# Loading w1 by SBUF rows (80 and 48 of 128) instead of by thirds of every row

## What is computed

```
# 1. linear attention with decay; B=4, H=8, S=768, D=48
cur = einsum('bhd,bhe->bhde', u * k_t, v_t)
y_t = einsum('bhd,bhde->bhe', r_t, state + cur)
state = w * state + einsum('bhd,bhe->bhde', k_t, v_t)
# 2. soft mixture of experts; x is 3072 x 384, phi 384 x 32, E=8 experts of 4 slots
logits = x @ phi
d = softmax over tokens;  c = softmax over slots
slot_input = (d.T @ x)                       # 8 x 4 x 384
slot_out[e] = relu(slot_input[e] @ w1[e]) @ w2[e]   # w1[e] 384 x 1024, w2[e] 1024 x 384
x = c @ slot_out
# 3. feed-forward; w_in 384 x 2048, w_out 2048 x 384
out = elu(x @ w_in) @ w_out
```

## Time and profile before

| what | value |
|---|---|
| median of 3 runs | 394.32 us (394.05 to 395.26) |
| profiled execution | 392.18 us |
| its span | 390.4 us |
| PE busy | 374.2 us, 96% |
| PEclk | 9 in all 40 slices |
| DMA queue of SP | 82368 packets, 50.21 MB, 43.1% of 16 engines |

### The profile page before, as it was taken

One profiled execution on the slowest core, in us unless ns is written; L12 is line 12 of the kernel. 1 busy time (PEld: TensorE's weight loads), 2 busy tenths in 40 slices (PEclk: granted clock), 3 DMA queues, 4 the chain that ended last, 5 costly groups with the idle time before them and its releaser, 6 DMA issues.

```text
span 390.4 us, 11439 instructions
## 1 busy us (share of the span) xinstructions
PE 374.2 (96%) x4373; PEld 333.0 (85%) x4373; DVE 267.6 (69%) x512; ACT 219.6 (56%) x498; POOL 103.3 (26%) x136
## 2 busy tenths in 40 slices
PE   6898999999889999999999999999999999999996
PEld 3787898989775454589999999999999999999996
DVE  4787788778767620699867767667777667776671
ACT  2896778777772131588564446444644464455441
POOL 7797777777640000355200000000000000000000
PEclk9999999999999999999999999999999999999999
DMA  7989899999999999920020002000200020002002
GB/s 152 254 151 186 199 234 233 227 255 254 235 303 426 430 432 403 373 64 2 0 83 1 2 0 81 0 0 0 81 0 0 0 81 0 0 0 82 2 2 81
DMA packets 87280, 51.80 MB, mean 133 GB/s; under 512 B 77776, under 2 KB 83024, under 8 KB 85200
## 3 DMA queue, kind: packets, MB, share of 16 engines
q1 hardware_dynamic: 82368, 50.21, 43.1%
q10 hardware_dynamic: 4880, 1.16, 1.4%
HBM read 45.86 MB, written 4.72 MB: 130 GB/s over the span
## 4 chain that ended last, share of the span: by engine, by line
PE 79%; DMA 10%; SPq 3%; issue 3%; ACT 3%; DVE 1%; POOL 1%; DVEq 0%; POOLq 0%; ACTq 0%
PE psum L976 17%; PE psum L978 17%; PE psum L977 17%; PE psum L911 6%; DMA w_out_raw<-in_moe_w_out_dram 4%; PE psum L603 4%; DMA r_raw<-in_r_dram 3%; PE psum L643 3%; PE psum L826 3%; PE psum L686 3%; PE psum L667 2%; PE psum L656 2%; PE psum L696 2%; DMA v_sb<-in_v_dram 1%; PE psum L703 1%
## 5 line engine op out<-in xcount | busy, mean ns | idle before, releaser
L978 PE MATMUL psum<-w_out_hi,elu_lo 128*128 128x384 f32 x372 | 125.8, 338 | 0.0
L976 PE MATMUL psum<-w_out_hi,elu_hi 128*128 128x384 f32 x372 | 125.7, 338 | 0.0
L977 PE MATMUL psum<-w_out_lo,elu_hi 128*128 128x384 f32 x372 | 125.3, 337 | 0.0
L1405 ACT ACTIVATE exp_h<-psum 128x512 f32<-128x512 f32 x96 | 57.6, 600 | 97.3 <-PE psum L911 97.0
L1246 DVE SCALAR_TENSOR_TENSOR elu<-psum,neg_part 128x512 f32<-128x512 f32 x96 | 66.3, 690 | 57.1 <-ACT neg_part L1392 57.1
L977 PEld LDWEIGHTS psum<-w_out_lo,elu_hi 128*128 128x128 f32 x372 | 69.8, 188 | 3.9
L976 PEld LDWEIGHTS psum<-w_out_hi,elu_hi 128*128 128x128 f32 x372 | 70.4, 189 | 0.0
L978 PEld LDWEIGHTS psum<-w_out_hi,elu_lo 128*128 128x128 f32 x372 | 69.9, 188 | 0.0
L1238 DVE TENSOR_TENSOR elu_lo<-elu,elu_hi 128x512 fp32r<-128x512 f32 x96 | 66.3, 691 | 0.6
L1280 ACT ACTIVATE scores<-ident_wide,bonus 128x128 f32<-128x128 f32 x192 | 58.8, 390 | 5.0 <-DVE bonus L1028 4.9
L1392 ACT ACTIVATE neg_part<-exp_h 128x512 f32<-128x512 f32 x96 | 60.0, 626 | 1.7 <-DVE elu L1246 1.3
(11 more groups left out here) (155 smaller groups left out, 403.6 us busy)
## 6 DMA issues: line engine op xcount, KB each, us to landing
w<-in_moe_w_dram SPq DMA_DIRECT2D x8, 1536.0 KB, 13.6
w_sb<-in_moe_w_dram SPq DMA_DIRECT2D x8, 1024.0 KB, 6.3
out_dram<-out_sb SPq DMA_DIRECT2D x24, 192.0 KB, 1.9
w_sb<-in_moe_w_dram SPq DMA_DIRECT2D x8, 512.0 KB, 6.2
w_out_raw<-in_moe_w_out_dram SPq DMA_DIRECT2D x4, 768.0 KB, 15.7
r_raw<-in_r_dram SPq DMA_DIRECT2D x12, 192.0 KB, 3.2
r_raw<-in_r_dram SPq DMA_DIRECT2D x24, 96.0 KB, 3.4
w_in_sb<-in_moe_w_in_dram SPq DMA_DIRECT2D x1, 2304.0 KB, 19.4
```

Source lines behind the costliest of these rows:

```text
L976: pe.matmul(acc, hi, w_out_hi[:, f, :], start=(f == 0), stop=False)
L977: pe.matmul(acc, hi, w_out_lo[:, f, :], start=False, stop=False)
L978: m = pe.matmul(acc, lo, w_out_hi[:, f, :], start=False, stop=(f == KF2 - 1))
L1405: act.activation(exp_h[:, f % 2, :], banks[4 + f % RING][:, :], ACT.Exp).then_inc(exp_done, 1)
```

## The change

The pieces of w1 are cut across the other dimension. In the chunks a piece is now SBUF rows 0 to 79, whole (80 x 12 KB, 960 KB); at the head and in the last chunk it is rows 80 to 127, whole (48 x 12 KB, 576 KB). Number and order of the DMAs and every wait stay as they are; `w1_sb` and its readers are unchanged.

```diff
-            def load_w1(experts, thirds):
+            def load_w1(experts, rows):
 
                 for e in experts:
-                    sp.dma_start(w1_sb[:, e * KD + thirds.start:e * KD + thirds.stop, :], w1_dram[e][:, thirds, :]
-                                 ).then_inc(w1_loaded, 16)
+                    sp.dma_start(w1_sb[rows, e * KD:(e + 1) * KD, :], w1_dram[e][rows, :, :]).then_inc(w1_loaded, 16)
...
                     if not first and not last:
-                        load_w1([2 * (c - 1) + g], slice(0, 2))
+                        load_w1([2 * (c - 1) + g], slice(0, 5 * P // 8))
                     if last and g == 0:
-                        load_w1(range(2, E), slice(2, KD))
+                        load_w1(range(2, E), slice(5 * P // 8, P))
...
-            load_w1(range(2), slice(2, KD))
+            load_w1(range(2), slice(5 * P // 8, P))
```

## The result

The changed kernel takes 424.76 us (median of 6 runs, 421.82 to 425.31), the kernel before 394.19 us in the same comparison: the ratio is 1.080, 95% interval 1.074 to 1.085. The prediction said 413 us, within 393 to 424. The direction was right, and so was the reason given for it, that rows matter; the loss is 30.6 us, not 18.7, and just outside the range.

What follows compares the result with a forecast made beforehand. The prediction took the DMA queue, from the chunks' first load to w_out, to bound the feed-forward's start. Last chunk +11.2, chunks +6.0 and +0.5, head +1.0 gave +18.7 us on 394.3: 413 us, range 393 to 424.

Steps and rivals of the forecast that it cites:

- What bounds the kernel: From the chunks' first load to w_out: the feed-forward starts when the DMA queue has been worked off.
- Rows matter: Loads of w1 covering fewer SBUF rows run slower than their bytes, +18.7 us in sum; chance 0.62.
- The G_T moves: Sign from the kernel before: SBUF-to-SBUF moves on 32 rows, whose packets took 1.7 times as long as their bytes.
- Theory 1: Rows share fixed paths into SBUF; a load is as slow as the path with the most rows.
- Last chunk, +11.2: Six 48-row pieces of w1 in the last chunk take 19.9 us against 8.7, delaying w_out's landing by +11.2 us.
- the factor for 48 rows: In the last chunk and at the head, 48-row loads take 2.4 times their time by bytes, at most 2.67.
- Chunks, +6.5: 80-row pieces in the chunks: six from 48 us on cost +6.0 us, the two before 48 us +0.5 us.
- Head, +1.0: Two 48-row pieces delay chunk 1's k and r loads by 3.7 us, mostly covered by free DMA time: +1.0 us.
- What is late next: In the last chunk w1 lands late and PE stands about 5 us at line 826, not adding to the sum.
- Rows don't matter: Rival for all w1 pieces: only bytes and packet length count, 392.9 to 394.3 us; chance 0.20.
- The engines even it out: Rival: free engines go on to other loads; chunks lose nothing, last chunk only part, +2 to +7 us; chance 0.12.
- Worse than the bound: Rival: head pieces make PE stand in chunk 1, or more than two engines meet on rows: over 424 us; chance 0.06.

Runs made afterwards that it cites:

- e2_alternate: Changed kernel, but w1 cut into every second row (even rows in the chunks, odd rows at the head and in the last chunk): 395.05 us, ratio to before 1.0055.
- e1_halves: Changed kernel, but w1 cut into rows 0-63 in the chunks and rows 64-127 at the head and in the last chunk: 420.84 us, ratio to before 1.070.
- e6_mirror: Changed kernel, but odd experts mirrored: rows 48-127 in the chunks, 0-47 at the head and in the last chunk: 421.26 us, ratio to before 1.071.
- e4_first_two: Kernel before, with whole rows for w1's experts 0 and 1 alone (80 in chunk 1, 48 at the head): 401.23 us, ratio 1.0225.
- e5_last_six: Kernel before, with whole rows for w1's experts 2 to 7 alone (80 in chunks 2 to 4, 48 in the last chunk): 417.55 us, ratio 1.064.
- e3_quarter: Changed kernel, but w1 cut into rows 0-95 in the chunks and rows 96-127 at the head and in the last chunk: 414.12 us, ratio to before 1.053.

## Why the prediction was right in kind and wrong in size

**What bounds the kernel.** Right. The loss appears in full at w_out's landing (29.7 us), and nothing behind it moved.

**Rows matter (0.62).** Right, and shown: e2_alternate and e1_halves differ only in which rows, and by 25.8 us. The G_T moves had been a true sign, although they don't read HBM. That the rows act where they are written, and not where they are read, rests on those moves and on w_out's 396 GB/s, not on an experiment of its own. Theory 1 is the rule that the prediction weighed, "SBUF — State Buffer", section "Door 1: The DMA port swizzle", of the Trainium skill. The runs agree with it where it says that rows 0-63 reach no more ports than rows 0-31 do: 768 KB on 64 rows against 384 KB on 32 took 7.7 against 4.7 us as a pair. They agree, too, with the section "Can I just issue two DMAs to hit both halves?" of the same page of the Trainium skill, by which two loads on different halves don't run beside each other: e6_mirror saved a tenth. They don't test the page's map row by row.

**Last chunk, +11.2, measured +17.5.** The step that failed most is the factor for 48 rows. It was set at 2.4, with 2.67 as its upper bound; measured were 1.37 us a packet, 2.95 times w2's. The bound was the ratio of the rows, 128 to 48; counting 8 rows on the fullest path for either load gives the same number. It supposes that a full path is never idle. The beat of three in the DMA row looks like engines released in groups, which would leave gaps; why the bound was passed was not tested. The factor makes 24.2 us instead of 19.9, +4.3 us. The other 2.0 us are not resolved; the chunk piece ahead of the six was issued only 2.9 us before them (117.10 and 119.95 us) instead of 4.2 and was itself slower, so more of it stood in line ahead of them. The Trainium skill's figures, too, had given 21.7 us for the six by the estimate in the prediction; measured were 24.2, and the measurement decides.

**Chunks, +6.5, measured +7.9.** An interval between pieces grew from 9.66 to 10.98 us on average, +1.3 instead of +1.0, but the last one, to the six pieces, shrank from 4.2 to 2.9 us: from the third piece's issue to the six it is +5.1 us, where the prediction had +6.0. v's landing behind the piece, 6.8 us, was forecast as 6.5 or more. What was wrong is that the two pieces before 48 us would find cover: they cost 2.8 us together, not 0.5 (first to third issue 23.55 us instead of 20.73). e4_first_two shows the same with the other six as before, 23.5 us.

**Head, +1.0, measured +4.3.** The same error in a larger form. I took some 4 us of idle DMA time as cover, but that time did not lie where the delayed loads were: POOL stood 4.4 us for k in the changed kernel, and PE stood 3.66 us in the middle of one group of matmuls at line 642, at 23.4 us. e5_last_six, with the head as before, has its first chunk piece back at 35.67 us. The other traces follow the rows of the two pieces at the head: 36.95 us with 96-127 (e3_quarter), 37.16 with every second row (e2_alternate), 41.51 with 64-127 (e1_halves), 42.44 with 80-127 and 0-47 (e6_mirror). PE's stop comes with the late ones: 3.1 us in e4_first_two, 5.0 in e1_halves and 4.5 in e6_mirror, always after 22 of 32 matmuls; e2_alternate, e3_quarter and e5_last_six have none there. Beside it the granted clock fell: 0.83 in the window from 13.5 to 34 us, where it had been 1.00; one group of eight matmuls at line 602, 1.02 us long at the full clock, took 1.90 us after PE's stop. No experiment here separates the stop's share from the late k's.

**What is late next.** Right in kind: line 825 started at w1's landing (151.77 us instead of 128.0), and that did not add to w_out's delay. But PE stood only 0.85 us there, not about 5, since it had already stood 7.48 us in line 702, which the prediction did not have.

**Rivals.** "Rows don't matter" is out by e1_halves against e2_alternate, and what e2_alternate measured, 395.05 us, is the case in which only bytes and packets count: there the longer packets brought nothing that can be seen. "The engines even it out" is out by e6_mirror. "Worse than the bound", given 0.06, is what the time says, by the head, which is one of the ways it named, and by a price above the bound. Whether the latter is its other way, more than two engines meeting on the same rows, was not tested by itself; packets of 1.37 us would fit three, if an engine takes neighbouring rows.

## What to carry to other kernels

A load over part of SBUF's rows can cost as much as one over all 128: 576 KB on 48 neighbouring rows took as long as 1536 KB on 128. If a tensor must be cut by rows, cut it by a step (every second, every fourth row), or cut along the free dimension; with every second row the pace was 411 GB/s. Some idle DMA time on average is no cover for a delayed load; look for who wants that load, and whether the idle time lies ahead of it.

## What the runs showed of the hardware that was not expected

**TensorE can stop for its own instructions behind slow data loads.** In the changed kernel PE stood 7.48 us between two matmuls of one group (line 702, after 17 of 32), with nothing in the program to wait for. PE's timeline:

```profile
132.65 0.73 PE L702 MATMUL psum<-y_T,phi_sb 128*32 128x128 f32 x17
140.86 1.08 PE L702 MATMUL psum<-y_T,phi_sb 128*32 128x128 f32 x15 [7.48 <-issue]
```

The DMA view from 133 to 141.5 us has one packet on a queue of its own for instructions, in the middle of w1's 48-row pieces:

```profile
q8 instruction: 1, 0.02, 1.1%
```

The chain of the kernel before breaks the same group at the same matmul, but for 0.08 us:

```profile
119.07 0.65 PE psum L703 x17
119.72 0.08 issue
119.80 0.64 PE psum L703 x15
```

Stops at this place came in every kernel with neighbouring rows in the last chunk (7.2 us in e5_last_six, 6.7 in e6_mirror, 4.2 in e1_halves, 2.8 in e3_quarter), and of 0.9 us in e4_first_two, whose last chunk is as before; with every second row the group is unbroken. The kernel before's longest wait put down to issue on PE was 1.4 us. That the instructions come late because they pass through the same engines is inferred from these views; no run moved the instruction packet alone. Here the stop cost nothing at the end, since w_out was later still.

**More rows can be slower than all of them.** A pair of 80-row loads landed in 8.9 us and of 96-row loads in 9.8 us on average, of 128-row loads with more bytes in 7.8 us. How the engines share out 80 or 96 rows was not measured.
